# The second expert's second matrix loaded behind the first two gathers, its parts made later, and the first slot's products with the high part first

## The reference

```python
x = attention(q, k, v, s)                       # 4 x 8 heads, 576 tokens, head_dim 64; causal, biased by a cumulative sum
# mixture: D = 512, 8 experts, F = 1024
e = fresh argmax of x @ w_gate, or the previous token's expert where sigmoid(x @ w_local) >= 0.5
out = softmax(x @ w_gate)[e] * (relu(x @ w1[e]) @ w2[e])
# second block: conv over tokens (3 taps) and a gate
h = relu(out @ w_in); g = h * sigmoid(conv3(h)); result = g @ w_out
```

## Time and profile before

| what | value |
|---|---|
| median of 3 runs | 724.52 us (723.65 to 725.7) |
| the profiled execution | 725.15 us, its span 723.4 us |
| PE busy / DVE / POOL / ACT | 98% / 64% / 48% / 44% of the span |
| granted TensorE clock, mean | 0.995 of full speed |

### The profile page before, as it was taken

One profiled execution on the slowest core, in us unless ns is written; L12 is line 12 of the kernel. 1 busy time (PEld: TensorE's weight loads), 2 busy tenths in 40 slices (PEclk: granted clock), 3 DMA queues, 4 the chain that ended last, 5 costly groups with the idle time before them and its releaser, 6 DMA issues.

```text
span 723.4 us, 13465 instructions
## 1 busy us (share of the span) xinstructions
PE 711.8 (98%) x4181; PEld 587.3 (81%) x4181; DVE 464.8 (64%) x1088; ACT 315.9 (44%) x633; POOL 348.9 (48%) x453
## 2 busy tenths in 40 slices
PE   8999999999998999999999999999999999999998
PEld 6777767676687888888888888888999989899886
DVE  5778777788877455666657566575399747636610
ACT  4778787787612022232222232010488436435510
POOL 7668887878515465674827568051454420000000
PEclk8999999999999999999999999999999999999999
DMA  7888887885144668988789667631424430000011
GB/s 166 209 218 230 214 217 220 221 224 152 46 151 128 216 211 303 282 241 269 229 282 309 225 217 259 232 117 56 135 88 117 139 95 15 29 30 15 30 44 58
DMA packets 121143, 120.08 MB, mean 166 GB/s; under 512 B 64604, under 2 KB 89460, under 8 KB 120948
## 3 DMA queue, kind: packets, MB, share of 16 engines
q1 hardware_dynamic: 100932, 73.26, 35.5%
q10 hardware_dynamic: 16672, 34.69, 14.7%
q0 software_dynamic: 3472, 11.28, 5.6%
HBM read 89.50 MB, written 29.70 MB: 165 GB/s over the span
## 4 chain that ended last, share of the span: by engine, by line
PE 70%; DVE 1%; DMA 1%; issue 0%; ACT 0%; POOLq 0%; DVEq 0%; ACTq 0%
PE wide_bank L1388 19%; PE wide_bank L1751 14%; PE row_bank L1791 14%; PE row_bank L1405 10%; PE bank L1405 9%; PE bank L1354 1%; DMA x_slots<-x_rows,token_of 1%; PE wide_bank L1427 0%; PE bank L1720 0%; PE bank L1740 0%; PE row_bank L1740 0%; PE bank L1030 0%; PE bank L1731 0%; PE wide_bank L28 0%; PE row_bank L1731 0%
## 5 line engine op out<-in xcount | busy, mean ns | idle before, releaser
L916 POOL TENSOR_TENSOR ring<-raw_w,ring 128x2048 fp32r<-128x2048 f32 x28 | 128.7, 4619 | 91.1 <-ACT ring L906 91.1
L906 ACT ACTIVATE ring<-raw_w 128x2048 fp32r<-128x2048 f32 x30 | 55.8, 1909 | 195.8 <-DMA raw_w<-in_moe_w_dram 161.6
L1751 PE MATMUL wide_bank<-x_tr,ring 128*128 128x288 f32 x768 | 106.0, 296 | 0.0
L1751 PEld LDWEIGHTS wide_bank<-x_tr,ring 128*128 128x128 f32 x768 | 103.5, 188 | 1.1
L690 ACT ACTIVATE prob<-score,row_min 128x128 f32<-128x128 f32 (+2 forms) x144 | 83.4, 579 | 38.8 <-PE turn_ps L362 25.7
L1791 PE MATMUL row_bank<-ring,g_tr 128*128 128x512 f32 x432 | 100.1, 389 | 0.0
L1791 PEld LDWEIGHTS row_bank<-ring,g_tr 128*128 128x128 f32 x432 | 80.4, 188 | 16.1
L1854 DVE SCALAR_TENSOR_TENSOR conv<-h_pad,conv_col,conv 128x576 f32<-128x576 f32 x64 | 53.0, 828 | 51.0 <-ACT conv L1915 49.6
L252 POOL TENSOR_SCALAR bias<-ncum_row,cum_col 128x128 f32<-128x128 f32 (+3 forms) x128 | 66.8, 532 | 37.2 <-DVE row_min L551 33.4
L551 DVE CUSTOM_DVE_ANT_0 score<-score_ps,bias 128x128 f32<-128x128 f32 (+2 forms) x144 | 69.2, 513 | 20.8 <-issue 14.4
L1388 PE MATMUL wide_bank<-ring,xs_tr 128*128 (+1 forms) x312 | 75.0, 395 | 0.4 <-DVE xs_tr L1479 0.4
(11 more groups left out here) (257 smaller groups left out, 1127.8 us busy)
## 6 DMA issues: line engine op xcount, KB each, us to landing
raw_w<-in_moe_w_dram ACTq DMA_DIRECT2D x12, 2048.0 KB, 12.0
x_slots<-h_turn SPq DMA_DIRECT2D x84, 128.0 KB, 3.0
ncum_row<-cum_rows SPq DMA_DIRECT2D x15, 512.0 KB, 4.9
raw_w<-in_moe_w_dram SPq DMA_DIRECT2D x12, 512.0 KB, 4.1
h_turn<-h_sb SPq DMA_DIRECT2D x11, 512.0 KB, 5.8
h_turn<-x_slots SPq DMA_DIRECT2D x10, 512.0 KB, 7.4
ncum_tail<-cum_rows SPq DMA_DIRECT2D x32, 144.0 KB, 4.3
out_dram<-out_sb ACTq DMA_DIRECT2D x18, 256.0 KB, 2.0
```

The source lines that it names most:

```text
L906: nc.scalar.activation(high, whole, ACT.Copy).then_inc(high_ready, 1)
L916: nc.gpsimd.tensor_tensor(low, whole, high.bitcast(F32), ALU.subtract).then_inc(low_ready, 1)
L1751: last = nc.tensor.matmul(wide_bank[j % 2][:, half, 0:HALF], ring[:, 0, w, col:col + P], x2_tr[:, x, kb, at:at + HALF], start=kb == 0 and ...
```

## The change

SP issues the load of `w2[1]` not before the mixture's first store, but behind it and behind waits for the first two gathers. ACT makes that matrix's two high parts after the relu of slot 0, not before. DVE makes its low parts after `move_x(2)`, not before `move_x(1)`. POOL's memset that counts them stands behind 14 gathers, not 8. And the first 12 products of slot 0 wait for high and low parts of the tokens apart, in an order of their own (`hidden_first`).

```diff
--- before.py
+++ after.py
@@ -974,7 +974,6 @@
     def sync_route(sp):
         sp.wait_ge(logit_ready, B)
         sp.wait_ge(x_done, B * KD)
-        load_weights(sp, 1, 1, w2[1])
 
     def pool_early(pool):
         nc.gpsimd.memset(gates[:, :, P:P + 2 * (E + 1)], 0.0).then_inc(gates_zero, 1)
@@ -1256,6 +1255,9 @@
     def sync_experts(sp):
         sp.wait_ge(y_zero, 1)
         sp.dma_start(y_sorted[LAST:LAST + P, :], y_sb[:, :]).then_inc(last_zeroed, 16)
+        for s in range(2):
+            sp.wait_ge(slot_loaded[s], 16)
+        load_weights(sp, 1, 1, w2[1])
 
         def h_write(s):
             n, i = s % 2, s - BY_PE
@@ -1306,11 +1308,10 @@
             act.wait_ge(y_done, slots_upto(e - 2))
             load_weights(act, e % 2, 1, w2[e] if e < E else w_out)
 
-        high_parts(act, 1, 0, 1)
-
         for half in range(2):
             act.wait_ge(h_done, half + 1)
             nc.scalar.activation(h_sb[:, half * FH:(half + 1) * FH], h_bank[:, half, :], ACT.Relu).then_inc(h_ready, 1)
+        high_parts(act, 1, 0, 1)
         act.wait_ge(slot_ready, 1)
         first_matrix(2)
         high_parts(act, 0, 1, 0)
@@ -1325,11 +1326,12 @@
     def pool_experts(pool):
         gather_slots(pool, 4, 8)
 
+        pool.wait_ge(tokens_sorted, 2)
+        ahead = SLOTS - E + 2
+        gather_slots(pool, 8, 14)
         pool.wait_ge(second_low, PIECES // 2)
         nc.gpsimd.memset(counted[:, :], 0.0).then_inc(low_ready, PIECES // 2)
-        pool.wait_ge(tokens_sorted, 2)
-        ahead = SLOTS - E + 2
-        gather_slots(pool, 8, ahead)
+        gather_slots(pool, 14, ahead)
         low_parts(pool, 2, 0)
         gather_slots(pool, ahead, ahead + 2)
         for e in range(2, E):
@@ -1376,13 +1378,9 @@
             n = weights_of(s, 0) if loaded is None else loaded
             if s:
                 pe.wait_ge(xs_ready, s + 1)
-            elif 0 in halves:
-                pe.wait_ge(half_ready, 1)
             for half in halves:
                 above(pe, h_ready, 2 * s + (half - 1))
                 for kb in range(KD):
-                    if s == 0 and half == 0 and kb == KD // 2:
-                        pe.wait_ge(xs_ready, 1)
                     at = kb * F + half * FH
                     for a, b in PARTS:
                         last = nc.tensor.matmul(h_bank[:, half, :], xs_both[s % 2][:, a, kb, :],
@@ -1390,6 +1388,17 @@
                                                 start=kb == 0 and (a, b) == PARTS[0],
                                                 stop=kb == KD - 1 and (a, b) == PARTS[-1])
                 last.then_inc(h_done, 1)
+
+        def hidden_first():
+            n = KD // 2
+            for side, (high_sem, ready_sem) in enumerate(((half_high, half_ready), (xs_high, xs_ready))):
+                for a in range(2):
+                    pe.wait_ge((high_sem, ready_sem)[a], 1)
+                    for kb in range(side * n, (side + 1) * n):
+                        for b in range(2 - a):
+                            last = nc.tensor.matmul(h_bank[:, 0, :], xs_tr[:, a, kb, :], ring[:, 0, b, kb * F:kb * F + FH],
+                                                    start=(side, a, kb, b) == (0, 0, 0, 0), stop=(side, a, kb) == (1, 1, KD - 1))
+            last.then_inc(h_done, 1)
 
         def output(s, blocks=range(KF), loaded=None, ends=False):
             n = weights_of(s, 1) if loaded is None else loaded
@@ -1431,7 +1440,7 @@
         turn_first_x()
         keep_running(nc, wide_bank[1][:, 0, :], identity, 2)
         pe.wait_ge(low_ready, PIECES // 2)
-        hidden(0, (0,), 0)
+        hidden_first()
         turn_x(1)
         hidden(0, (1,), 0)
         pe.wait_ge(slot_ready, 1)
@@ -1547,16 +1556,16 @@
             V.tensor_copy(y_both[s % 2][:, :], y_banks[s % 2][:, :]).then_inc(y_ready, 1)
 
         move_first_x()
-        for piece in range(PIECES // 2, PIECES):
-            dve.wait_ge(high_ready, PIECES + piece + 1)
-            whole, high, low = piece_of(1, piece)
-            V.tensor_tensor(low, whole, high.bitcast(F32), ALU.subtract).then_inc(second_low, 1)
         move_x(1)
         move_h(0)
         vector_weights(dve, then)
         dve.wait_ge(last_zeroed, 16)
         relu(1)
         move_x(2)
+        for piece in range(PIECES // 2, PIECES):
+            dve.wait_ge(high_ready, PIECES + piece + 1)
+            whole, high, low = piece_of(1, piece)
+            V.tensor_tensor(low, whole, high.bitcast(F32), ALU.subtract).then_inc(second_low, 1)
         move_y(0)
         move_h(1)
         relu(2)
```

## The result

| | median | runs | ratio to before (95%) |
|---|---|---|---|
| before | 723.54 us (722.68 to 725.7) | 20 | |
| changed | 728.24 us (721.79 to 730.39) | 20 | 1.0047 (1.0032 to 1.0062) |

The change makes the kernel slower, by 0.47% or 4.7 us. Its runs lie in two groups: 6 of 20 took 721.8 to 723.8 us (their middle 722.5), 14 took 726.1 to 730.4 (their middle 729.2). Before had one group of 3 us. The profiled execution took 728.63 us, its span 726.9; it is one of the fourteen.

The account below looks back on a forecast made before the run. TensorE, never idle from 260 to 510 us, was taken as the bound, so slot 0's earlier start is kept: 1.25 + 0.40 = 1.65 us off 724.52 gives 722.9 us, range 721.8 to 724.2.

Parts of the forecast that it names:

- Gather 0: Slot 0's start: with no load in flight, the gather lands after 3.8 us instead of 5.06, gaining 1.25 us.
- instruction packet: Instruction-queue packet at 216.6 to 219.7 us, expected again during gather 0, adding 0.4 to 1.0 us to a clean 3.5.
- The fillers: Identity products ahead of gather 0's use on TensorE, ending at 217.83, so no landing under 3.19 us could show.
- The high part first: Slot 0's first product waits for the high part only and starts at 220.85 instead of 221.25, gaining 0.40 us.
- The subtractions' cover: DVE's two moved subtractions delay slot 0's copy 1.1 us; slot 1's turned parts have 4.3 us cover, cost 0.
- The slower rival: Moved load lands after 16.8 us, subtractions hold slot 1's parts, TensorE waits; 22 us would give 728; chance 4%.
- ACT and SP: ACT free long before its next load at 246.98, SP's next store after 240; the moved instructions cost 0.
- Gathers and POOL: Gathers share DMA with the moved load; POOL's idle time and the third expert's 2.4 us cover absorb delays, cost 0.
- The sum: Whole kernel: 1.25 us from gather 0 plus 0.40 from the product order, 1.65 us gained, giving 722.9 us.
- The chances: Measured outcome: 0.22 faster by over 0.3%, 0.73 within, 0.05 slower by over 0.3%.
- 6% for a thin cover that breaks: Third expert's low parts over 2.4 us late, TensorE waits 0.2 to 1.2 us at 271.00: 723.1 to 724.1; chance 6%.

Follow-up runs that it names:

- e1: The kernel before with only the new order of slot 0's first 12 products (`hidden_first`); 723.02 us, ratio 0.9993.
- e2: The changed kernel with only the load of `w2[1]` back at its old place, before the zero store; 722.96 us, ratio 0.9988.
- e7: e2 with the last two early gathers held until TensorE has finished eight halves; 723.23 us, ratio 1.0002.
- e11: e4 with the old order of slot 0's first products and their old waits; 723.41 us, ratio 0.9994.
- e4: The changed kernel with 3 of the 19 early gathers issued later, among the experts; 722.09 us, ratio 0.9983.
- e9: The changed kernel run again unaltered for a second profile; 727.55 us, ratio 1.0039, its profiled run 723.60 us.
- e12: The changed kernel with 2 of the 19 early gathers moved behind the third expert's low parts; 722.41 us, ratio 0.9982.

## Why the prediction was wrong

**Gather 0** (forecast 3.8 us, a gain of 1.25): 3.64 us, a gain of 1.4 over the profile of before. The number is right, but e1, e2 and e7, with the load at its old place, had 4.59, 4.72 and 4.81, against which the gain is 1.0 to 1.2. And 0.3 us of the 3.8 stood for an instruction packet that no longer meets the gather: with the load at its old place it passes while gather 0 is in flight (before, e1, e2, e7), here it passes between 212.0 and 213.07, before the gather's issue, and in none of the other profiles with the load moved does it fall into gather 0's time. By the prediction's own figures that makes 3.5 us and a gain of 1.55; seven of these profiles had 3.5 to 3.7. That the forecast of 3.8 came this close owes something to luck. The fillers never bound.

**The high part first** (0.40 us): 1.50 to 1.11 us, 0.39. Right; e1 and e11 give it alone.

**The subtractions' cover** (4.3 us, of which 1.1 used): right. The load landed at 228.9, so the high parts ended at 232.6, just before the forecast's 233; subtractions 233.23 to 237.7, no gap behind them. The slower rival, whose place was here, didn't come near: the load took 10.6 us, not 16.8.

**ACT and SP** (cost 0): the moved instructions cost nothing themselves, but the step looked only at what stands next on each queue up to 247 us, not at the exchange on SP nor at the load on ACT that meets it.

**Gathers and POOL** ("three gathers of two to three microseconds' delay fit in", "Cost 0, and thin"): this is the step that failed, twice over. The size: where two to three microseconds of delay were put down, the last early gather went out 5.2 us later by the wall and 6.8 later counted from the issue of gather 0. The prediction priced a load that runs with gathers from the load's side (1.3 us for three, 0.9 for two more; the load of 243.54 took 10.6 us instead of 10.4), but not the other side, what one gather loses (7.9 instead of 3.3), nor that with two in flight each loss is passed on. It used the slowest landing for gather 2 alone, and found that one in time. The question: it asked whether the gathers would be through before POOL and TensorE wanted them, and they just were: the third expert's low parts began at 257.93 instead of 255.84 in e4, in time by some 0.4 us here and late by 0.25 in e9. It did not ask what the delayed gathers would now run beside. They came into the path of slot 3's write, whose reads then fell behind a 2 MB load with a lead of only 0.83 us. Each of these covers could be read in the trace of before, and none was.

**The sum**, 1.65 us: where the exchange is left alone, something of this size is gained, though less by the medians. e4 and e12 came to 722.09 and 722.41, 1.2 and 1.3 us under the kernel before by their ratios, with intervals from 0.6 to 2.0; the changed kernel's six undisturbed runs have their middle at 722.5, 1.0 under before. That these times even lie below the forecast's 722.9 is because the three runs it started from had a median 1.0 us above that of the twenty (724.52 for 723.54). In the other fourteen runs 6.7 us go on top. The profile confirms it beside e4, which started at the same time (first product at 217.87 in both): TensorE's last stretch before the second block is 6.6 us later (first product on `y_tok` at 513.21 for 506.61), and 0.4 us more is lost there, where the chain waits for a late `y_tok`.

**The chances**: slower had 5%, of which 4% for another mechanism. The 6% for a thin cover that breaks named the right engine, POOL, and the wrong victim, and priced it without the clock: an idle time of 3.3 us on TensorE cost 6.5.

The best versions, e4 and e12, keep the change and issue two or three gathers later. They beat both kernels: 0.17 and 0.18% under before, intervals 0.9974 to 0.9992 and 0.9972 to 0.9991. It is a gain below the 0.3% taken as telling, though neither interval includes 1.

## What to carry to other kernels

When a large transfer is moved among a chain of small ones, follow the whole chain to its last member and list every transfer of other queues that it now meets, with the lead each of those had: the cover that broke here was 0.83 us wide, some 40 us behind the moved load. Price a wait of TensorE with the products behind it at the lower clock, not by its own length. And look at each run, not the median alone: two groups 6.7 us apart were a race between transfers, and the gain sought was there in the one of them.

## What was not expected of the hardware

- A write of 512 KB took 2.6 us with no gather in its way, 3.2 to 3.3 us with one issued 0.5 us before it, and 4.0 to 4.3 us with one issued 0.75 to 1.07 us before it.
- Four 128 KB reads took 2.5 to 3.3 us ahead of a 2 MB load (before, e4); where the load was issued among them, the last two took 6.5 and 8.0 us; where it was issued with the first, 9.7 us in the median (3.7 the first, 12.2 the last).
- In a wait of 3.3 us on TensorE the granted clock fell to 0.50 and stayed there for 6.8 us, some 6 of them behind the wait; 24 products took 8.53 us, with fillers in place of the wait 5.74.
